# Staging expert 0's weights through two slots instead of their own eighth

## The reference

```python
# attention, B=2, H=8, S=768, D=64, block 32, window 16
k_sum = k.reshape(B, H, nb, block, D).max(axis=3)
v_sum = v.reshape(B, H, nb, block, D).mean(axis=3)
scores_l = where(|i - j| < window, scale * q @ k.T, -1e9)
scores_s = scale * q @ k_sum.T + log(block)
a = softmax(concat(scores_l, scores_s));  x = a @ concat(v, v_sum)
# mixture, N=1536 tokens, D=512, E=8 experts, F=1024
e = argmax(cos(x, expert_emb) / tau);  gate = softmax(...)[e]
out = gate * (relu(x @ w1[e]) @ w2[e])
# rational MLP, 512 -> 2048 -> 512
h = x @ w_in;  g = P3(h) / (1 + |b0||h| + |b1|h^2 + 1e-6);  out = g @ w_out
```

## Time and profile before

| | |
|---|---|
| median of the runs | 668.95 us |
| the profiled execution's own time | 668.95 us |
| its span | 667.4 us |
| PE busy | 639.8 us (96%) |
| DVE busy | 473.4 us (71%) |
| ACT busy | 405.3 us (61%) |
| POOL busy | 156.5 us (23%) |
| chain that ended last: PE | 79% |
| chain that ended last: DMA | 8% |
| DMA bytes | 87.07 MB |

### The profile page before, as it was taken

The page is one execution under the profiler, slowest core; times in us unless marked ns, Lnnn a source line. Parts: engine busy times, 40 slices in busy tenths (PEclk is TensorE's granted clock), DMA queues, the critical chain, the costliest instruction groups (busy, mean ns, idle before and its releaser), DMA issues.

```text
span 667.4 us, 11274 instructions
## 1 busy us (share of the span) xinstructions
PE 639.8 (96%) x3377; PEld 533.1 (80%) x3377; DVE 473.4 (71%) x944; ACT 405.3 (61%) x762; POOL 156.5 (23%) x198
## 2 busy tenths in 40 slices
PE   5999999987999999999999999999999999999996
PEld 4689999865878787888888888888888888888885
DVE  6877776676569753432134478999898898898886
ACT  6577777554468753443145468776676666676663
POOL 3668968742010023101012001010020000200000
PEclk9999999998999999999999999999999999999999
DMA  8978998597759973375145102001010000100001
GB/s 292 260 175 219 231 218 207 193 329 283 268 194 384 335 255 52 82 252 185 32 156 206 51 21 59 1 17 31 17 63 2 17 0 1 41 24 0 1 1 63
DMA packets 57610, 87.07 MB, mean 130 GB/s; under 512 B 33016, under 2 KB 33032, under 8 KB 56400
## 3 DMA queue, kind: packets, MB, share of 16 engines
q1 hardware_dynamic: 50656, 66.10, 31.8%
q0 software_dynamic: 6448, 20.22, 9.2%
q10 hardware_dynamic: 448, 0.02, 0.0%
HBM read 63.54 MB, written 13.74 MB: 116 GB/s over the span
## 4 chain that ended last, share of the span: by engine, by line
PE 79%; DMA 8%; DVE 4%; ACT 4%; issue 3%; POOL 1%; SPq 0%; DVEq 0%; ACTq 0%; POOLq 0%
PE bank L1770 20%; PE bank L1785 19%; PE bank L1733 12%; PE bank L1712 11%; PE bank L1484 8%; DMA raw_late<-in_moe_w_dram 4%; PE bank L1558 3%; PE bank L1584 2%; ACT weights L871 2%; DVE weights L1230 2%; PE bank L1586 2%; PE bank L1607 2%; DMA kraw<-in_k_dram 1%; DMA xg<-x_by_slot 1%; DMA KWs<-KW 1%
## 5 line engine op out<-in xcount | busy, mean ns | idle before, releaser
L1770 PE MATMUL bank<-X2T,weights 128*128 128x512 f32 x576 | 143.1, 397 | 0.0
L1785 PE MATMUL bank<-weights,G 128*128 128x512 f32 x576 | 139.4, 391 | 1.8 <-DVE G L1230 1.8
L1785 PEld LDWEIGHTS bank<-weights,G 128*128 128x128 f32 x576 | 108.0, 188 | 26.5 <-DVE G L1230 2.6
L1770 PEld LDWEIGHTS bank<-X2T,weights 128*128 128x128 f32 x576 | 107.7, 188 | 24.9
L1733 PE MATMUL bank<-weights,HT 128*128 (+1 forms) x456 | 112.7, 402 | 2.4 <-DVE HT L1230 2.4
L1712 PE MATMUL bank<-weights,XT 128*128 (+1 forms) x432 | 108.7, 400 | 4.2 <-issue 1.6
L1733 PEld LDWEIGHTS bank<-weights,HT 128*128 128x128 f32 x456 | 85.3, 190 | 22.7 <-issue 3.3
L1712 PEld LDWEIGHTS bank<-weights,XT 128*128 128x128 f32 x432 | 79.6, 188 | 23.8 <-issue 4.2
L923 ACT ACTIVATE qd<-bank,coef 128x512 f32<-128x512 f32 x48 | 33.0, 688 | 75.7 <-PE bank L1770 75.6
L1230 DVE TENSOR_TENSOR HT<-bank,HT 128x512 fp32r<-128x512 f32 x38 | 24.5, 685 | 65.3 <-ACT HT L951 64.5
L1230 DVE TENSOR_TENSOR weights<-raw_late,weights 128x2048 f32 (+2 forms) x20 | 41.4, 2076 | 24.2 <-ACT weights L871 24.1
(11 more groups left out here) (239 smaller groups left out, 1103.0 us busy)
## 6 DMA issues: line engine op xcount, KB each, us to landing
raw_early<-in_moe_w_dram SPq DMA_DIRECT2D x14, 1024.0 KB, 7.0
raw_late<-in_moe_w_dram SPq DMA_DIRECT2D x14, 1024.0 KB, 9.5
KWs<-KW SPq DMA_DIRECT2D x48, 184.0 KB, 4.1
y_in_order<-yo POOLq DMA_DIRECT2D x19, 256.0 KB, 2.9
xg<-x_by_slot POOLq DMA_DIRECT2D x18, 256.0 KB, 5.6
raw_in_low<-in_moe_w_dram SPq DMA_DIRECT2D x8, 512.0 KB, 4.3
qraw<-in_q_dram SPq DMA_DIRECT2D x12, 256.0 KB, 4.8
kraw<-in_k_dram SPq DMA_DIRECT2D x2, 1024.0 KB, 9.9
```

The costliest lines, as they stand in the source:

```text
L1770: last = T_.matmul(bank[6 + f % 2][:, :], W[:, 0, wa, kc * F2 + f * P:kc * F2 + (f + 1) * P], X2T[c % 2][:, xa, kc * C_TOK:(kc + 1) * C_TO ...
L1785: last = T_.matmul(bank[tt][:, :], G[:, f % 2, ga, tt * P:(tt + 1) * P], W[:, 1, wa, f * DM:(f + 1) * DM], start=(f == 0 and n_ == 0), sto ...
```

## The change

The eight pieces of expert 0 are no longer loaded into the place of their low parts. They pass through two slots of 4 KB per partition, which lie in `x_all`: slot 0 in tiles 7 and 8, slot 1 in tiles 9 and 10. This has four consequences in the code.

- A load of piece j waits until piece j - 2 has been split (`w0_ready`). Pieces 0 and 1 are issued in SP's iteration T = 2, piece T - 1 in iteration T from T = 3 on.
- POOL splits piece T - 3 in iteration T, from T = 3 to T = 10. `mean_v(2)` runs between `windows(3, 0)` and `windows(3, 1)`, no longer after `split_q(4)`.
- The scatters of tiles 0 to 2 are issued in POOL's iteration 10, those of tiles 3 to 5 in iteration 11; the last split is no longer behind them.
- `make_x(7)` waits until piece 6 is split and `make_x(9)` until piece 7 is.

```diff
-        in_low = Region(base + SLAB * 4).take("raw_in_low", [P, SLAB], F32)
-        raw0 = [in_low[:, j * CH // 2:(j + 1) * CH // 2] for j in range(2 * CHUNKS)]
+        raw0 = [x_all[:, NT - 5 + 2 * i:NT - 3 + 2 * i, :].rearrange("p t d -> p (t d)") for i in range(2)]
...
             def load_raw(j):
                 c, half = divmod(j, 2)
-                sp.wait_ge(kt_mm, KG * FILLS)
-                if c == CHUNKS - 1:
-                    sp.wait_ge(vmean_ready, KG)
+                if j >= 2:
+                    sp.wait_ge(w0_ready, j - 1)
+                else:
+                    sp.wait_ge(ks_mm, 1)
...
-                sp.dma_start(dst, src).then_inc(raw0_in[j], 16)
+                sp.dma_start(dst, src).then_inc(raw0_in[half], 16)
...
                 load_v(T)
-                if 0 <= T - 3 < 2 * CHUNKS:
-                    load_raw(T - 3)
+                if T == 2:
+                    load_raw(0)
+                    load_raw(1)
+                if 2 <= T - 1 < 2 * CHUNKS:
+                    load_raw(T - 1)
...
             def split_slab0(j):
                 if j == 0:
-                    pool.wait_ge(kmax_ready, KG)
-                pool.wait_ge(raw0_in[j], 16)
+                    pool.wait_ge(kt_mm, KG * FILLS)
+                    pool.wait_ge(vm_mm, 2)
+                pool.wait_ge(raw0_in[j % 2], 16 * (j // 2 + 1))
                 dst = W[:, 0, :, j * CH // 2:(j + 1) * CH // 2]
-                G_.tensor_copy(dst[:, HI, :], raw0[j]).then_inc(hi0_done, 1)
+                G_.tensor_copy(dst[:, HI, :], raw0[j % 2]).then_inc(hi0_done, 1)
...
             windows(3, 0)
-            windows(3, 1)
-            split_q(4)
             mean_v(2)
 
+            SCATTERS = {10: (0, 1, 2), 11: (3, 4, 5)}
...
-            for T in range(4, NT):
-                windows(T, 0)
+            for T in range(3, NT):
+                if T > 3:
+                    windows(T, 0)
                 windows(T, 1)
                 if T + 1 < NT:
                     split_q(T + 1)
-                    split_slab0(T - 4)
-            for T in range(NT - 6):
-                scatter(T)
-            split_slab0(2 * CHUNKS - 1)
+                if T - 3 < 2 * CHUNKS:
+                    split_slab0(T - 3)
+                for t in SCATTERS.get(T, ()):
+                    scatter(t)
...
             def make_x(T):
                 dve.wait_ge(rsum_done, T + 1)
                 dve.wait_ge(pv_mm, PAIRS * (T + 1))
+                if T in (NT - 5, NT - 3):
+                    dve.wait_ge(w0_ready, 2 * CHUNKS - (1 if T == NT - 5 else 0))
```

More of the change, by code:

```diff
@@ L246, in moe_mlp_kernel @@
         raw_in = [sem(f"raw_in{i}") for i in range(CHUNKS)]
-        raw0_in = [sem(f"raw0_in{j}") for j in range(2 * CHUNKS)]
+        raw0_in = [sem(f"raw0_in{i}") for i in range(EARLY_SLOTS)]
         hi0_done, w0_ready = sem("hi0_done"), sem("w0_ready")
@@ L450, in load_raw @@
                 c, half = divmod(j, 2)
-                sp.wait_ge(kt_mm, KG * FILLS)
-                if c == CHUNKS - 1:
-                    sp.wait_ge(vmean_ready, KG)
+                if j >= 2:
+                    sp.wait_ge(w0_ready, j - 1)
+                else:
+                    sp.wait_ge(ks_mm, 1)
                 if c < 2:
-                    dst = raw0[j].rearrange("p (k f) -> p k f", f=F)
+                    dst = raw0[half].rearrange("p (k f) -> p k f", f=F)
                     src = w1_v[0, :, c * HALFK + half:c * HALFK + half + 1, :]
@@ L458, in load_raw @@
                     at = (c - 2) * HALFF + half * HALFF // 2
-                    dst = raw0[j].rearrange("p (k f) -> p k f", f=DM)
+                    dst = raw0[half].rearrange("p (k f) -> p k f", f=DM)
                     src = w2_v[0, :, at:at + HALFF // 2, :]
-                sp.dma_start(dst, src).then_inc(raw0_in[j], 16)
+                sp.dma_start(dst, src).then_inc(raw0_in[half], 16)
             load_k(0)
@@ L603, in split_slab0 @@
                 if j == 0:
-                    pool.wait_ge(kmax_ready, KG)
-                pool.wait_ge(raw0_in[j], 16)
+                    pool.wait_ge(kt_mm, KG * FILLS)
+                    pool.wait_ge(vm_mm, 2)
+                pool.wait_ge(raw0_in[j % 2], 16 * (j // 2 + 1))
                 dst = W[:, 0, :, j * CH // 2:(j + 1) * CH // 2]
-                G_.tensor_copy(dst[:, HI, :], raw0[j]).then_inc(hi0_done, 1)
+                G_.tensor_copy(dst[:, HI, :], raw0[j % 2]).then_inc(hi0_done, 1)
                 pool.wait_ge(hi0_done, j + 1)
-                G_.tensor_tensor(dst[:, LO, :], raw0[j], dst[:, HI, :].bitcast(F32), ALU.subtract)\
+                G_.tensor_tensor(dst[:, LO, :], raw0[j % 2], dst[:, HI, :].bitcast(F32), ALU.subtract)\
                   .then_inc(w0_ready, 1)
```

## The result

| | before | after |
|---|---|---|
| median of 15 runs each, one chip | 670.83 us | 677.46 us |
| lowest and highest | 667.24, 674.27 | 672.95, 680.76 |
| the profiled execution's own time | 668.95 us | 679.31 us |
| its span | 667.4 us | 677.8 us |

The ratio after to before is 1.0076, with a 95% interval of 1.0053 to 1.0098. It is the recorded ratio, over more runs than the table has (32 of after), and so not the quotient of the table's medians, which would be 1.0099. The change costs some 5 us. The prediction said 670.9 us (ratio 1.003) with 673.5 as its upper end: the direction of the main term was right, and the time is outside the range. On the prediction's base of 668.95 us the ratio gives 674.0 us, which is outside it too.

A forecast was written before the change was run, and what follows sets the result against it. PE was taken to bound attention (busy 58.10 of 58.60 us), with POOL and the DMA rings close behind. 668.95 + 2.3 (tile 4's windows) - 0.4 (given back) = 670.85, so 670.9 us; range 668.3 to 673.5.

The forecast's parts named there:

- Tile 4's windows, the main term: One split (3.43 us) ahead of windows(4, 0) on POOL makes the swap late; unit 16 starts 2.3 us late (1.3 to 2.9).
- "Nothing, barely" at unit 12: Tile 3's first swap, behind loads 0 and 1, lands at 51.5 to 52.1 us, wanted at 52.18: no loss.
- Rival 1: PE's pause at unit 16 also lowers its clock, costing 1.7 us more: 672.6 us; chance 0.18.
- Given back, 0.4: After tile 4, fewer POOL waits for weight loads return 0.4 us of attention's 1.2 us of small waits (0 to 1.2).
- windows(3, 1) and load_v(3): At tile 3, both come later but still in time, load_v(3) by about 0.6 us: no loss.
- second stall at tile 5: Tile 5's swap lands at 70.1 us, wanted at 70.9 after the shift: no second stall.
- rival 2: DVE waits at make_x(7) for split 6 near 104 us, costing 2 us: 672.9 us; chance 0.15.
- the eighth split and the early scatters: Late in attention, the eighth split leaves its place behind six scatters and three scatters precede windows(11): zero for both.
- Rival 3: Tile 4's swap lands below about 3.6 us, stall 1.3, 1.5 given back: 668.75 us, not slower; chance 0.15.

The follow-up runs named there:

- e4: The kernel before with POOL's new order and the loads as early as in the change, but no slots and its own scatters: 675.61 us, ratio 1.0099.
- e6: The changed kernel without the five adds of mean_v(2), 5.46 us of POOL work: 672.06 us, ratio 1.0019.
- f3: The kernel before with 3.4 us of extra POOL work, one split's size, between mean_v(2) and windows(4, 0): 681.34 us, ratio 1.0078.
- f2: The changed kernel with loads 0 and 1 between tile 3's swaps and without mean_v(2)'s five adds: 681.22 us, ratio 1.0036.
- g4: The same kernel as f2, run a second time: 680.73 us, ratio 1.0041.
- g2: The changed kernel again, unchanged, on another chip: 681.89 us, ratio 1.0079.
- e1: The changed kernel with its first six scatters moved back behind the last tile's windows: 675.74 us, ratio 1.0085.
- e7: The kernel before with only the loads of pieces 0 and 1 moved ahead of tile 3's first swap: one run, 672.04 us.
- f1: The changed kernel with loads 0 and 1 issued between tile 3's two swaps instead of ahead of both: 682.72 us, ratio 1.0065.
- f4: The kernel before with only the weight loads moved early, POOL's order untouched: 681.53 us, ratio 1.0065.
- e8: The changed kernel with 18 extra transposes on PE ahead of its wait at unit 16, and the s_read wait moved earlier: 675.64 us, ratio 1.0066.
- e5: The changed kernel's slots and waits, but first four pieces loaded and split as late as before, two splits in tile 8, scatters last: 674.73 us, ratio 1.0081.
- e2: The changed kernel with tile 4's windows and swap ahead of the first split and of load 2: 675.59 us, ratio 1.0082.
- g1: The kernel before again, unchanged, on another chip: 677.95 us, ratio 1.0008.

## Why the prediction was wrong, point by point

**Tile 4's windows, the main term: mechanism right, size too small.** e4 (order and loads alone give the loss), e6 (less POOL work takes most of it away by the ratio) and f3 (one split's worth of work gives it in before) show it; f2 and g4 point the same way, within the noise. f3 reproduces the working's times to 0.1 us. In after the same chain was 1.8 us later at SP: POOL began it at 45.52 instead of the 44.26 that I took over from before, and the first issue of the swap took 1.08 us instead of 0.50. In e4 and g2 that issue took 0.50, and the landing 5.3 and 4.9 us in its place. So unit 16 was later than unit 10 by 3.7 us in after, 2.8 in e1, 4.0 in e4, 3.8 in g2, where the forecast was 2.3 and its upper end 2.9. This term was too small by 1.4 us in after, and by 0.5 to 1.7 in the four.

**"Nothing, barely" at unit 12: wrong.** It lost 1.4 us in after, 1.0 in e1, 1.1 in e4 and 1.6 in e7 (nothing in g2). The two loads took 2.08 us of SP's queue in after where I had 1.2. But it was not a term of the sum, since f1 takes it away and unit 16 stays as late.

**The rings: missing from the working.** I gave the swap 4.4 us to land (3.4 to 5.0) and asked only when it was issued. In after it took 4.5. With the loads early, issues at 56.2, 56.4, 56.8 and 57.5 us (e6, f4, f2, g4) were all usable only at 63.95 to 64.6, after 6.7 to 8.2 us. So with POOL earlier, and the loads as early as in the change, unit 16 would still have been late. That the ring share stands at 1.00 in the earlier trace rows was in my text, and I drew nothing from it for the swap.

**The clock: left out of the sum, and it came.** Rival 1 had a chance of 0.18 and a price of 1.7 us. After lost 1.49 us so, e1, f3, f4 and g4 the same, f1, f2 and g2 from 2.3 to 3.1; e4, e6 and e8 nothing. The Trainium skill (TensorE: Matmul & The Clock Gate, "HAM oscillation — how this bites in real kernels") says that waiting on a DMA between matmul groups can throttle the clock again; after agrees, at a PE that was full on both sides of the pause, which I had held against it; e4 shows the same pause without it. On the chips where before takes 670 us, 13 of 32 runs of after had a mean granted clock under 0.994, and 6 of 46 of before. The means are 674.63 (over) and 678.05 us (under) for after, 670.19 and 673.83 for before. So on the same side of 0.994 after is 4.2 to 4.4 us slower, and the larger share of low-clock runs adds 0.41 x 3.4 - 0.13 x 3.6 = 0.9 us; the two make up the difference of the means, 5.4 us. This split does not price the pause at unit 16: a mean over a whole run doesn't say where the clock was low, and the profiled execution of after, at 0.987, has both that pause and the standstill near 125 us.

**Given back, 0.4: wrong.** POOL's 9.3 us of waits for weights turned into 9.7 us more of waits for queries (24.5 against 14.8), under PE's cover both. From unit 20 to unit 44 after gains nothing (5.70 and 5.85). The bound was misread too: before's first scores of units 16 and 44 stand at 60.38 and 118.74, so the seven pitches are 58.36 us and their excess is 0.96, in three tiles (0.30, 0.49 and 0.18), not 1.2 mostly in one.

**Right as forecast.** windows(3, 1) and load_v(3) made nothing late; no second stall at tile 5; no wait of DVE for POOL near 104 us (rival 2 did not come in after; e5 shows that its mechanism and its price were right); the eighth split and the early scatters moved nothing in after (e1). Rival 3 needed a landing under 3.6 us, and no run showed one at unit 16.

**The sum again with measured sizes.** 3.7 at unit 16 without the clock and 1.5 for the clock are 5.2 us above a profile like before's: 668.95 + 5.2 = 674.2, a ratio of 1.0078. This is worked out after the fact, from one profile. It is close to the median loss, and not a proof that the loss is made of these two in every run: f3's ratio is larger than its two parts, and the profile of e6 is later than its ratio. The failed step is the size of the tile 4 term (3.7 us measured, 2.3 in the sum) and the choice to leave the clock out of the sum (1.5 us measured, 0 in the sum). The range was too narrow because the two were judged apart, though the second comes behind the first and adds to it.

## What to carry to other kernels

When work is put ahead of a producer on an engine that has been busy without a break, take the start of that chain as a range too, and add to any forecast stall of a full PE the clock that such a stall can cost, as one case. A transfer that is wanted in 5 us must not be costed by its usual landing time if the same edit moves a megabyte or more in front of it: read the ring share of that stretch, and where it is at 1.00 add the backlog. In this kernel, work without slack could not be placed better by moving it (e2, e5); it had to become less (e6).

## What the runs showed of the hardware

- A 184 KB swap between two SBUF tiles landed in 4.3 us with the rings as in before (f3) and in 6.7 to 8.2 us behind early weight loads at a ring share of 1.0 to 1.3 (f4, g4). Issued at 56.41 in f4 and at 60.09 in after, it was usable at 64.59 in both.
- A pause of PE of 2.1 us between full stretches was followed by 4 us with a granted clock of 0.52 and 0.63 (after), and a pause of 2.7 us was not (e4). With 18 extra transposes in the pause it stayed at 1.00 (e8).
- DVE and ACT stand still for some 3 to 7 us between 120 and 132 us in nine of 18 profiles (3.99 in after, 3.64 in g1, 6.91 in f4), released by nothing that the profile names in most of them, while the first six scatters are under way or just behind them. Mostly it goes with the chip: all eight profiles on two of them, none of the eight on two others. What it is stays open.
- Two of four chips ran the same kernel in 670.4 and 670.6 us, two in 678.1 and 677.5. The ratio of after to before was the same, within its interval, where before took 671 and where it took 678 us: 1.0076 and 1.0079.
